# Attention and two MLPs on one core: where shift and reciprocals stand, what is turned, and the order of the first second products

## What is computed

```python
# attention: 2 batches, 8 heads, 1152 keys, head dimension 64; queries pooled in twos to 576
q_pool = q.reshape(B, H, S // 2, 2, D).mean(axis=3)
scores = scale * q_pool @ k^T ; scores -= max over keys
attn = exp(scores) ; attn = attn / (sum(attn) + 1e-9) ; out = attn @ v
# rows of all heads side by side: 1152 tokens x 512
h = x @ w_in          (512 -> 2048); g = P(h) / (Q(h) + 1e-6), P cubic, Q from |h| and h^2
x = g @ w_out
xn = x / rms(x) * rms_g
y = (silu(xn @ w_gate) * (xn @ w_val)) @ w_out2      (512 -> 1536 -> 512)
```

## Time and profile before

| | |
|---|---|
| timed runs, median | 707.93 us (706.84 to 708.24) |
| the profiled execution | 710.97 us, span 709.2 us |
| TensorE busy | 681.6 us (96%) |
| VectorE busy | 528.8 us (75%) |
| GpSimd busy | 438.0 us (62%) |
| ScalarE busy | 411.7 us (58%) |
| mean granted TensorE clock | 0.988 |

### The profile page before, as it was taken

The page is one execution under the profiler, slowest core; times in us unless marked ns, Lnnn a source line. Parts: engine busy times, 40 slices in busy tenths (PEclk is TensorE's granted clock), DMA queues, the critical chain, the costliest instruction groups (busy, mean ns, idle before and its releaser), DMA issues.

```text
span 709.2 us, 11780 instructions
## 1 busy us (share of the span) xinstructions
PE 681.6 (96%) x3940; PEld 631.3 (89%) x3940; DVE 528.8 (75%) x1009; ACT 411.7 (58%) x855; POOL 438.0 (62%) x427
## 2 busy tenths in 40 slices
PE   8999997999799989799999999999999999999998
PEld 6999996999699979689999999989999999999996
DVE  6999996899699986889989989988664444444442
ACT  5787785778487766988888788873521111111110
POOL 5885887579578998798978888866543512000000
PEclk9999999899999999999999999999999999999999
DMA  8675737473746532011011101111220200000012
GB/s 230 189 217 108 211 80 204 125 196 107 183 138 152 137 95 75 0 60 61 14 47 61 59 1 61 61 59 61 81 99 1 82 37 1 0 1 1 1 44 90
DMA packets 24380, 60.76 MB, mean 86 GB/s; under 512 B 3208, under 2 KB 5776, under 8 KB 24208
## 3 DMA queue, kind: packets, MB, share of 16 engines
q1 hardware_dynamic: 24048, 59.87, 29.0%
q10 hardware_dynamic: 288, 0.33, 0.2%
HBM read 43.78 MB, written 2.40 MB: 65 GB/s over the span
## 4 chain that ended last, share of the span: by engine, by line
PE 72%; POOL 8%; DMA 7%; DVE 5%; issue 3%; ACT 3%; SPq 1%; POOLq 0%; ACTq 0%; DVEq 0%
PE hb L837 29%; PE ob L888 21%; PE sc L744 7%; PE sc L752 5%; PE misc L766 4%; PE tb L837 3%; PE pv_ps L766 3%; DMA o_part<-o_sb 3%; DMA recip_rows<-recip 2%; DMA r_row<-recip_rows 2%; DVE neg_part L1119 1%; DVE pt_lo L1130 1%; POOL kqB L526 1%; POOL o_part L596 1%; POOL num L708 1%
## 5 line engine op out<-in xcount | busy, mean ns | idle before, releaser
L954 ACT ACTIVATE pt_hi<-sc 128x384 fp32r<-128x384 f32 x216 | 90.8, 493 | 50.5 <-PE sc L752 50.0
L1130 DVE TENSOR_TENSOR pt_lo<-sc,pt_hi 128x384 fp32r<-128x384 f32 x216 | 107.0, 549 | 13.3 <-ACT pt_hi L954 12.8
L1119 DVE TENSOR_REDUCE neg_part<-sc 128x1 f32<-128x384 f32 x216 | 107.9, 548 | 11.9 <-PE sc L744 9.3
L888 PE MATMUL ob<-wo_hi,gt_hi 128*128 128x512 f32 x252 | 99.9, 396 | 3.7 <-issue 2.8
L888 PE MATMUL ob<-wo_hi,gt_lo 128*128 128x512 f32 x252 | 99.6, 395 | 0.0
L888 PE MATMUL ob<-wo_lo,gt_hi 128*128 128x512 f32 x252 | 98.7, 392 | 0.0
L837 PE MATMUL hb<-xt_hi,wi_hi 128*128 128x384 f32 x280 | 95.0, 339 | 3.5 <-POOL xt_lo L611 1.9
L837 PE MATMUL hb<-xt_lo,wi_hi 128*128 128x384 f32 x280 | 94.5, 338 | 0.0
L837 PE MATMUL hb<-xt_hi,wi_lo 128*128 128x384 f32 x280 | 94.3, 337 | 0.0
L945 ACT ACTIVATE prob<-sc,neg_max 128x1152 f32<-128x1152 f32 x72 | 89.1, 1237 | 3.3 <-DVE neg_max L1123 3.3
L752 PE MATMUL sc<-ident,prob 128*128 128x128 f32 x648 | 84.7, 277 | 0.6 <-ACT prob L945 0.6
(11 more groups left out here) (161 smaller groups left out, 1730.2 us busy)
## 6 DMA issues: line engine op xcount, KB each, us to landing
wraw<-in_moe_w_out SPq DMA_DIRECT2D x7, 1024.0 KB, 5.0
krawB<-in_k SPq DMA_DIRECT2D x8, 576.0 KB, 3.8
qrawB<-in_q SPq DMA_DIRECT2D x8, 512.0 KB, 5.1
wraw<-in_moe_w_in SPq DMA_DIRECT2D x4, 1024.0 KB, 5.1
krawA<-in_k SPq DMA_DIRECT2D x7, 576.0 KB, 4.4
o_part<-o_sb SPq DMA_DIRECT2D x14, 288.0 KB, 7.8
qrawA<-in_q SPq DMA_DIRECT2D x7, 512.0 KB, 5.0
wraw<-in_moe_w_gate SPq DMA_DIRECT2D x3, 1024.0 KB, 5.2
```

Source lines behind the costliest of these rows:

```text
L888: ins = nc.tensor.matmul(ob[(m + 1) % 2][:], gt[i][:, f, P * t:P * t + P], wo[c % 2][j][:, f, :], start=f == 0 and n == 0, stop=f == CHUNK ...
L954: nc.scalar.activation(pt[0][:, 3 * c:3 * c + 3, PT_COL[i]:PT_COL[i] + P], src, ACT.Copy).then_inc(pt_hi, 1)
L1119: nc.vector.tensor_reduce(neg_part[:, s, c:c + 1], sc[s][:, c, 0:KBANK], AX.X, ALU.max, negate=True).then_inc(part_done, 1)
L1130: nc.vector.tensor_tensor(pt[1][:, kt, col], src, pt[0][:, kt, col].bitcast(F32), ALU.subtract).then_inc(pt_lo, 1)
```

## The change

Four things are altered.
- SyncE, pairs 1 to 6: `shift` and `rows_of_recip` of pair h-1 go between the loads of A and the loads of B; both value loads follow one another.
- Reciprocals: VectorE makes them of the 128x9 sums, in tile 0 behind the low parts (for the last pair behind tile 4's low parts, and ahead of tile 8's); TensorE turns the reciprocals in tile 2 ahead of the values product, into columns 384 to 511 of the bank `misc` (for the last pair `pv_ps` in tile 5, and a score bank in tile 8); ScalarE copies them to `recip_t`, and SyncE sends that.
- The values product of the last group, and ScalarE's copy of it, go from behind unit 0 to behind unit 1, the copy now after `last_hi(2)`.
- Second products 0 and 1 both stand behind unit 7: three of the four units of both, then the fourth of both, each waiting only for the unit's own low part. None stands behind unit 8.

```diff
@@ SyncE @@
             def rows_of_recip(h, par):
-                sp.wait_ge(recip_done, h + 1)
-                sp.dma_start(recip_rows[par], recip[0:TILES, par]).then_inc(row_out, 16)
+                sp.wait_ge(recip_out, h + 1)
+                sp.dma_start(recip_rows[par], recip_t[0:TILES, par]).then_inc(row_out, 16)
...
                 load_kq(0, h + 1)
+                if not is_first(h):
+                    shift(h - 1, 1 - par, n)
+                    rows_of_recip(h - 1, 1 - par)
                 sp.wait_ge(k_split[1], h * 2 + 2)
                 sp.wait_ge(q_split[1], h * 4 + 4)
                 load_kq(1, h + 1)
                 sp.wait_ge(m_split, h * 4 + 4)
                 load_mixed(h + 1)
-                sp.wait_ge(v_split[0], h * 2 + 2)
-                load_v(0, h + 1)
+                for x in range(2):
+                    sp.wait_ge(v_split[x], h * 2 + 2)
+                    load_v(x, h + 1)
...
-                else:
-                    shift(h - 1, 1 - par, n)
-                sp.wait_ge(v_split[1], h * 2 + 2)
-                load_v(1, h + 1)
-                if not is_first(h):
-                    rows_of_recip(h - 1, 1 - par)
                 mixed_keys(0, h + 1)
@@ TensorE @@
+                    if g == 1 and not is_first(h):
+                        pe.wait_ge(recip_out, h)
+                    if g == 2 and is_last(h):
+                        pe.wait_ge(recip_out, PAIRS)
...
+            def turn_recip(n, par, t0=0, t1=TILES):
+                ins = nc.tensor.transpose(recip_bank(n)[0:t1 - t0], recip[:, par, t0:t1], ident[:])
+                ins.then_inc(recip_turned, 1)
...
+                    if i == 2 and not is_first(h):
+                        pe.wait_ge(recip_done, h)
+                        pe.wait_ge(o_evac, h * 4)
+                        turn_recip(0, 1 - par)
...
-                    if i == 2 and not is_first(h):
-                        pe.wait_ge(sums_done, h)
-                        pe.wait_ge(pt_lo, h * 27 + 7)
-                        turn_sums(sums_bank(s), 1 - par, 0, TILES)
...
-            def second_product(c, t):
+            def second_product(c, t, parts=range(CHUNK)):
...
-                if t % BT == 0:
+                if t % BT == 0 and m > 0:
                     pe.wait_ge(g_lo, UNITS * c + CHUNK * (t // BT + 1))
...
-                for f in range(CHUNK):
+                for f in parts:
+                    if m == 0:
+                        pe.wait_ge(g_lo, f + 1)
...
-                if u == 0:
+                if u == 1:
                     pv(3, PAIRS - 1, 0, 2 * KEY_TILES)
...
-                for c, t in behind(u, 0):
-                    second_product(c, t)
+                if u == 2 * CHUNK - 1:
+                    for parts in (range(CHUNK - 1), [CHUNK - 1]):
+                        for t in range(2):
+                            second_product(0, t, parts)
+                elif u > 2 * CHUNK:
+                    for c, t in behind(u, 0):
+                        second_product(c, t)
@@ ScalarE @@
+            def recip_copy(n, count, slot, t0=0, t1=TILES):
+                act.wait_ge(recip_turned, count)
+                nc.scalar.activation(recip_t[0:t1 - t0, slot], recip_bank(n)[0:t1 - t0], ACT.Copy).then_inc(recip_out, 1)
...
+                    if i == 2 and not is_first(h):
+                        recip_copy(0, h, 1 - par)
+                    if is_last(h) and i == 5:
+                        recip_copy(PAIRS - 1, PAIRS, 1, *SUMMED[0:2])
+                    if is_last(h) and i == 8:
+                        recip_copy(PAIRS, PAIRS + 1, 2, *SUMMED[1:3])
...
-                if u == 0:
+                if u == 1:
+                    last_hi(2)
                     o_copy(3, PAIRS - 1)
-                    last_hi(2)
@@ VectorE @@
-            def recips(bank, count, slot, t0=0, t1=TILES):
-                dve.wait_ge(sums_t, count)
-                nc.vector.reciprocal(recip[0:t1 - t0, slot], bank[0:t1 - t0]).then_inc(recip_done, 1)
+            def recips(count, par, t0=0, t1=TILES):
+                dve.wait_ge(sums_done, count)
+                nc.vector.reciprocal(recip[:, par, t0:t1], sums_eps[:, par, t0:t1]).then_inc(recip_done, 1)
...
+                    if is_last(h) and i == 8:
+                        recips(PAIRS + 1, par, *SUMMED[1:3])
                     lo_parts(i, h, s)
+                    if i == 0 and not is_first(h):
+                        recips(h, 1 - par)
+                    if is_last(h) and i == 4:
+                        recips(PAIRS, par, *SUMMED[0:2])
```

More of the change, by code:

```diff
@@ L114, in build @@
         sums_eps = sbuf(top, "sums_eps", [P, 2, TILES])
-        recip = sbuf(top, "recip", [P, 3, P])
+        recip = sbuf(top, "recip", [P, 2, TILES])
+        recip_t = sbuf(top, "recip_t", [P, 3, P])
         att = ExitStack()
@@ L264, in build @@
         sums_done = sem("sums_done")
-        sums_t = sem("sums_t")
         recip_done = sem("recip_done")
+        recip_turned = sem("recip_turned")
+        recip_out = sem("recip_out")
         raw_w = sem("raw_w")
@@ L385, in last_rows @@
                 t0, t1 = SUMMED[n], SUMMED[n + 1]
-                sp.wait_ge(recip_done, PAIRS + n)
-                sp.dma_start(recip_rows[1, t0:t1], recip[0:t1 - t0, 1 + n]).then_inc(tail_out[n], 16)
+                sp.wait_ge(recip_out, PAIRS + n)
+                sp.dma_start(recip_rows[1, t0:t1], recip_t[0:t1 - t0, 1 + n]).then_inc(tail_out[n], 16)
                 sp.wait_ge(tail_out[n], 16)
@@ L851, in first_product @@
                         pe.wait_ge(tail_lo, nb)
+                if u == 1:
+                    pe.wait_ge(pt_lo, 27 * PAIRS)
                 if u == CHUNK:
-                    pe.wait_ge(recip_done, PAIRS + 1)
+                    pe.wait_ge(recip_out, PAIRS + 1)
                 if f == 0 and mlp2 and c == NC1:
@@ L872, in first_product @@
                 ins.then_inc(s1_done, 1)
-            def second_product(c, t):
+            def second_product(c, t, parts=range(CHUNK)):
                 m = TILES * c + t
-                if t == 0:
+                if t == 0 and parts[0] == 0:
                     key = ("out", c) if c < NC1 else ("out2", c - NC1)
                     pe.wait_ge(w_split, 8 * at[key] + 8)
-                if t % BT == 0:
+                if t % BT == 0 and m > 0:
                     pe.wait_ge(g_lo, UNITS * c + CHUNK * (t // BT + 1))
@@ L883, in second_product @@
                     pe.wait_ge(acc_done, m - 1)
-                elif m == 0:
+                elif m == 0 and parts[0] == 0:
                     pe.wait_ge(o_evac, 4 * PAIRS)
-                for f in range(CHUNK):
+                for f in parts:
+                    if m == 0:
+                        pe.wait_ge(g_lo, f + 1)
                     for n, (i, j) in enumerate(((0, 0), (1, 0), (0, 1))):
@@ L889, in second_product @@
                                                start=f == 0 and n == 0, stop=f == CHUNK - 1 and n == 2)
-                ins.then_inc(s2_done, 1)
+                if parts[-1] == CHUNK - 1:
+                    ins.then_inc(s2_done, 1)
             pe.wait_ge(warm, 1)
@@ L1114, in _, with row_max @@
             split_first(dve)
-            def row_max(i, h, s, between=None):
+            def row_max(i, h, s):
                 n = (h * 9 + i) * 3
@@ L1119, in row_max @@
                     nc.vector.tensor_reduce(neg_part[:, s, c:c + 1], sc[s][:, c, 0:KBANK], AX.X, ALU.max, negate=True).then_inc(part_done, 1)
-                    if c == 0 and between:
-                        between()
                 dve.wait_ge(part_done, n + 3)
@@ L1138, in pair @@
                     s = (par + i) % 2
-                    between = None
-                    if i == 3 and not is_first(h):
-                        between = lambda: recips(sums_bank(1 - s), h, 1 - par)
-                    if i == 6 and is_last(h):
-                        between = lambda: recips(sums_bank(1 - s), PAIRS, 1, *SUMMED[0:2])
                     if i + 1 < TILES:
-                        row_max(i + 1, h, 1 - s, between)
+                        row_max(i + 1, h, 1 - s)
                     elif not is_last(h):
                         row_max(0, h + 1, 1 - s)
-                    if i == 8 and is_last(h):
-                        recips(sc[0][:, 0, 0:P], PAIRS + 1, 2, *SUMMED[1:3])
+                    if is_last(h) and i == 8:
+                        recips(PAIRS + 1, par, *SUMMED[1:3])
                     lo_parts(i, h, s)
+                    if i == 0 and not is_first(h):
+                        recips(h, 1 - par)
+                    if is_last(h) and i == 4:
+                        recips(PAIRS, par, *SUMMED[0:2])
             def tokens_lo(t):
```

18 lines of the change are left out of this document (8 added, 10 removed).

## The result

The changed kernel takes 700.12 us (median of 4 executions, 698.44 to 701.49), the kernel before 708.09 beside it (706.84 to 709.2): ratio 0.9887, 95% interval [0.986, 0.9914]. It is faster, by 1.1%, which is little more than half of what was forecast: 694.0 was the number, and the result lies 0.1 us past 700.0, the end of the range. The profiled execution took 700.05 us with a span of 698.3.

What follows compares the result with a forecast made beforehand. Clean pairs were held bound by TensorE and VectorE at once, two long pairs by a late shift. From 710.97 us, 13.34 + 2.25 + 1.65 came off and 0.95 on: 694.7, taken as 694.0, range 688.5 to 700.0.

Steps and rivals of the forecast that it cites:

- Shift earlier: SyncE's order: idle and half clock of the two long pairs both go, 7.53 + 5.81 = 13.34 us.
- 0.1 us a pair: Clean pairs: gain taken for shorter waits at ScalarE's copy of output group 0.
- a slow shift: Rival at 699.5 us: with first half's loads in flight, shift lands late and 0.9 us a pair stays; chance 0.09.
- late loads: Rival at 699 us: odd pairs' loads 1 to 3 us late, two or three pairs, some half clock; chance 0.11.
- a slower kernel: Rival: second half's loads land so late that GpSimd holds TensorE, about 718 us at a Z+28 landing; chance 0.03.
- The reciprocal: VectorE, tile 0: 0.15 us instead of 0.93, with an added wait; gain 0.35 us a pair, bounds nothing and 0.9.
- The 698 us: Time by the skill's costs: old reciprocal only 0.21 us, its removal saving next to nothing against the added wait.
- Last pair: Ahead of the first MLP product: both GpSimd gaps go, 1.65 us (bounds 0.55, 1.65); start moves 17.24 us in all.
- First second products: First MLP: 0.75 us gained, 1.7 lost to half clock behind a 4.4 us wait; net 0.95 slower (bounds -2.1, +2.9).
- The chain term: First MLP: chain to unit 7's low part 0.75 us shorter, as ScalarE gets unit 1 sooner (bounds 0, 2.1).
- the quarter that I took off: Timed runs lie 3.0 us below the profiled one; a quarter of that taken off 694.7 gave 694.0 us.
- The high end of the sum: Upper bound, 699.3 us, for ends that can occur together: 710.97 - 13.34 - 0.55 + 2.2.

Runs made afterwards that it cites:

- the shift alone: The kernel before with only SyncE's new order, shift and rows of reciprocals ahead of the second half's loads: 697.9 us, ratio 0.9851.
- the reciprocal one tile later: The changed kernel with VectorE's reciprocal behind the low parts of tile 1 instead of tile 0: 696.47 us, ratio 0.9841.
- the two placements: The changed kernel with 32 or 96 unused bytes a partition, so that later tensors lie further: 702.21 us with 32, 701.02 with 96.
- GpSimd's products earlier: The reciprocal one tile later, plus GpSimd's third and fourth split of w_out moved behind num 0 and 1: 694.37 us, ratio 0.9793.
- the kernel with 416 bytes: "Unit by unit" with 416 unused bytes, so that later tensors lie 512 bytes further than in the kernel before: 690.68 us, ratio 0.9738.
- unit by unit: "GpSimd's products earlier" with the fourth second product waiting for each unit's own low part instead of all four: 690.48 us, ratio 0.9725.
- the last kernel: "Unit by unit" with GpSimd's w_in and w_out splits still later and SyncE's w_out load behind the last rows' sends: 693.82 us, ratio 0.977.

## Why the prediction was wrong

The forecast for the span was 16.3 us less; the profile has 10.9 less (709.2 to 698.3). The step that failed is the reciprocal's: a wait of VectorE was added on the engine that paces the pairs, and the prediction let the cheaper reciprocal more than make up for it. Beside it three terms were mis-sized or missing. Step by step:

*Shift earlier: right.* 13.34 us was to go and has gone, idle and half clock both, and the kernel with the shift alone has no long pair either. "0.1 us a pair" for the shorter waits at the same copy was too little, as the shift alone made the clean pairs 29.83 on average, from 30.05. The queue behind it was no hindrance: GpSimd's idle times from pair 1 to the last name only TensorE, loads of half A (1.9 us in all) and issue, none a load of half B. The rivals of a slow shift, of late loads and of a slower kernel are out; that two of them had 699.5 and 699 us, close to what was measured, is chance.

*The reciprocal: the step that failed.* The wait that I added came as described, with 0.65 us of idle. The next reduction starts 0.72 us late (133.44 = Z+0.48, before at Z-0.24), where 0.74 was said. The failed step is what follows from it, "then two tiles of 3.1", "gain 0.35 us a pair". I let the delay of the wait be made up by the missing 0.93 us and took the rest as a gain. The two tiles without the old reciprocal took 3.36 and 3.05 us instead of 3.58 and 3.53, so they gave 0.7 us, and tile 2 starts 0.70 late; nothing is left. The three kernels say: 29.83 with the old reciprocal and no new wait, 29.91 with the new one and the wait, 29.25 with the new one and no wait. So the new reciprocal is worth 0.58 us a pair, and the wait costs 0.66. The lower bound that I gave for this term, nothing, is what came, or 0.08 us less than nothing; over five pairs to the last but one's Z it costs 1.4 us against the forecast. The duration, 0.21 for an assumed 0.15 us, is a small part of it. By the Trainium skill ("Vector Engine (DVE) Microarchitecture Reference", section 5.2: some 1.04 ns per column and 75 ns each) the new form would take an estimated 0.084 us and the old one 0.21. The traces have 0.21 and 0.93. The 698 us that I had worked out from it and set aside, with the saved reciprocal bringing next to nothing beside the wait, was nearer than my 694.0, but by luck: the old reciprocal did take 0.93 us, and with the wait out of the way 0.58 a pair comes back.

*Last pair: mis-sized, by the same wait.* The first MLP product moved by 15.0 us, 265.38 to 250.38, for 17.24 forecast: 1.4 of the missing 2.2 is the pair term up to pair 6's Z, the rest that pairs 6 and 7 gave 0.8 less than their 1.65. Both of GpSimd's gaps did close: it no longer waits for `r_row` in `two_heads`, and the 0.55 us ahead of the last heads are 0.1. But in pair 6 GpSimd takes up the queries of A at Z+4.52 (197.28), and before at Z+3.85; in the program it waits there for a values product of TensorE's, which comes later now. These 0.67 us are the reciprocal's wait again: with the reciprocal one tile later it is Z+3.85.

*First second products.* That TensorE would wait "4.4 us" for unit 7's low part and lose the clock behind it was right in place and kind: 3.88 us, clock 0.70 for 9.96 us. I took 1.7 us, and in this execution it is 2.74 (2.9 was the bound). But behind waits of 3.92, 3.84, 3.96 and 3.65 us, in the four other kernels with this wait (the reciprocal one tile later, the two placements, GpSimd's products earlier), the 36 products lose 1.3, 1.4, 1.6 and 1.5 us against the 7.25 that they take at a clock of 1.00. So 1.7 was a fair size, and about 1 us of this miss belongs to the one execution that was profiled. The chain term, -0.75, brought 0.2 (42.39 to 42.19), since GpSimd's first `num` was never waiting for the values product. It stood behind four `w_out` splits, as GpSimd's timeline of the changed kernel shows:

```profile
250.29 0.62 POOL L650 TENSOR_SCALAR wo_hi<-wraw 128x512 fp32r<-128x512 f32 x1
...
257.57 1.48 POOL L652 TENSOR_TENSOR wo_lo<-wraw,wo_hi 128x512 fp32r<-128x512 f32 x1
259.01 1.27 POOL L706 TENSOR_TENSOR num<-num,h 128x384 f32<-128x384 f32 x1
```

I had the splits in the argument for units 4 to 7 and did not look at what stood ahead of unit 0's `num`. Moving two of them gave 0.8 us.

*Pace of the second products: absent from the prediction.* In the chain 25 at 2.80 instead of 2.75 us, and others, make about 1.5 us (the stretch from the second product behind the fourth one's group to the end is 395.77 us, and was 394.22). A smaller tensor in a list of allocations was an edit to which I gave no cost.

*Sum of the misses:* pairs 1.4, last pair and first MLP product 0.8, chain 0.55, half clock 1.0, pace 1.5, together 5.3 of the 5.4 us by which the two spans differ from the forecast. Some 2 of them are the wait ahead of the reciprocal. The other 0.7 us between 694.0 and the measured 700.12 are the quarter that I took off for the base of the sum, which was one of the long executions. The high end of the sum, 699.3, did have both bad ends in it, nothing for the reciprocal and 2.9 for the clock. What carried the result past it is what the sum had at nothing or too high: the pace at 1.5, and the chain, which gave 0.2 where the high end counts 0.75; faster clean pairs and a last pair above its low bound took 1.1 of that back.

*Open:* by which rule addresses set the pace; why the gain from restoring it does not show in the timed runs, whose spread (688.24 to 695.37 us in the kernel with 416 bytes) is larger than 1.5 us; and what makes the loss behind the same wait 1.3 us in one execution and 2.7 in another.

## What to carry to other kernels

Move a transfer that someone waits for ahead of loads that nobody waits for yet: that one edit of SyncE's order was worth as much as the whole change. When an operation is moved and made cheaper, compare what it now waits for with what it saved, on the engine that paces the loop: 0.58 us of gain and 0.66 us of wait cancelled, and one tile later the gain was there. When TensorE must wait for the last of four inputs, let it do the products of the other three first, one by one: the wait fell from 3.65 to 1.60 us, and the clock behind it was granted at 1.00 instead of 0.63.

## What the hardware showed that I had not expected

- The same 12 products of 512 columns took 2.72 to 2.80 us and the same 12 of 384 columns 2.08 to 2.12, by where tensors lie in SBUF. Shifts that I count as 96 and 128 bytes gave 2.80 in more than half of the places, by 192 a mixture, by 512 the old 2.75.
- VectorE's reciprocal took 0.93 us for 9x128 and 0.21 for 128x9: its time went with the columns, not with the partitions.
- The clock did not follow the length of a wait alone: behind 1.82 and 1.90 us at the first MLP product, the 24 products took 6.03 us at a granted clock of 0.72 in the kernels with 512 bytes and with GpSimd's products earlier, behind 1.97 us in "unit by unit" 4.46 at 1.00. Ahead of the fourth second product 2.51 us were followed by 0.65 in "the shift alone", and 2.45 us by 1.00 in the last kernel. The chain and the timeline of "unit by unit":

```profile
246.89 4.46 PE hb L843 x24
```

```profile
246.89 0.45 PE L843 MATMUL hb<-xt_hi,wi_hi 128*128 128x384 f32 x1 [1.97 <-POOL xt_lo L611]
```
